# Attention, V's key spans of a unit: six transfers, alternately to the lower and the upper half of the partitions, in place of two

## The reference

```python
def _attn_ref(q, k, v):                  # batch 4, heads 8, seq 576, head_dim 64
    # 1: q, k, v averaged over groups of 4 tokens, full softmax attention on the 144 averages,
    #    each result repeated for its 4 tokens
    mask = np.abs(pos[:, None] - pos[None, :]) < factor        # factor = 4
    scores = np.where(mask, scale * np.matmul(q, k.transpose(0, 1, 3, 2)), -1000000000.0)
    out_local = np.matmul(softmax(scores), v)                  # 2: the seven nearest keys
    return out_up + out_local
def _moe_ref(x, w_in, w_out):            # 512 -> 2048 -> 512
    h = x @ w_in
    return (h * np.tanh(softplus(h))) @ w_out
def _moe2_ref(x, w_in, w_out, g_ln):     # 512 -> 1024 -> 512
    return (layernorm(h * softmax(h)) * g_ln) @ w_out          # h = x @ w_in
```

## Time and profile before

| | us |
|---|---|
| median of 3 runs | 689.77 |
| lowest and highest | 688.67, 690.86 |
| the profiled execution, first to last instruction | 686.9 |
| attention (start to the first product of the first feed-forward stage, L913) | 86 |

### The profile page before, as it was taken

One profiled execution on the slowest core, in us unless ns is written; L12 is line 12 of the kernel. 1 busy time (PEld: TensorE's weight loads), 2 busy tenths in 40 slices (PEclk: granted clock), 3 DMA queues, 4 the chain that ended last, 5 costly groups with the idle time before them and its releaser, 6 DMA issues.

```text
span 686.9 us, 12938 instructions
## 1 busy us (share of the span) xinstructions
PE 667.5 (97%) x5002; PEld 573.1 (83%) x5002; DVE 425.9 (62%) x747; ACT 326.0 (47%) x687; POOL 284.2 (41%) x342
## 2 busy tenths in 40 slices
PE   6998899999999999999999999999999999999998
PEld 5777778888999989989899988888778888888886
DVE  7998759555765557555544412555788566766671
ACT  5998773233543446543443211137464454535441
POOL 6999713020694636645000000576435543354100
PEclk9999999999999999999999999999999999999999
DMA  8999692000000000000100001012100000000001
GB/s 259 247 262 262 157 336 114 0 1 1 0 1 1 1 1 1 1 1 1 62 1 2 1 0 35 27 31 63 31 17 16 31 32 31 8 25 31 32 16 46
DMA packets 26085, 37.52 MB, mean 55 GB/s; under 512 B 2484, under 2 KB 12714, under 8 KB 26026
## 3 DMA queue, kind: packets, MB, share of 16 engines
q1 hardware_dynamic: 26026, 36.71, 18.0%
HBM read 31.98 MB, written 4.72 MB: 53 GB/s over the span
## 4 chain that ended last, share of the span: by engine, by line
PE 89%; POOL 3%; DVE 2%; issue 2%; ACT 1%; DMA 1%; SPq 0%; POOLq 0%; DVEq 0%
PE psum L961 29%; PE psum L913 16%; PE psum L1074 13%; PE psum L1051 12%; PE psum L947 12%; PE psum L1060 2%; PE psum L813 1%; POOL prob L676 1%; PE psum L845 1%; PE psum L893 1%; DVE so L1768 1%; PE psum L832 1%; POOL half_qk L649 1%; DMA qkT<-kT_dram 1%; POOL half_v L659 1%
## 5 line engine op out<-in xcount | busy, mean ns | idle before, releaser
L961 PE MATMUL psum<-ghi,whi 128*128 128x512 f32 (+1 forms) x320 | 118.2, 370 | 0.0
L961 PE MATMUL psum<-glo,whi 128*128 128x512 f32 (+1 forms) x320 | 118.1, 369 | 0.0
L961 PE MATMUL psum<-ghi,wlo 128*128 128x512 f32 (+1 forms) x320 | 117.7, 368 | 0.0
L1210 ACT ACTIVATE g_sb<-psum 128x512 f32<-128x512 f32 (+1 forms) x48 | 25.3, 527 | 135.5 <-PE psum L913 134.7
L1586 DVE CAST ghi<-g_sb 128x512 fp32r<-128x512 f32 (+1 forms) x48 | 24.0, 500 | 101.8 <-PE psum L961 86.7
L913 PE MATMUL psum<-xhi,whi 128*128 128x512 f32 (+1 forms) x256 | 85.6, 365 | 0.5 <-ACT g_sb L1210 0.3
L1591 DVE TENSOR_TENSOR glo<-g_sb,ghi 128x512 fp32r<-128x512 f32 (+1 forms) x80 | 66.3, 829 | 19.6 <-ACT ghi L1236 17.9
L961 PEld LDWEIGHTS psum<-ghi,wlo 128*128 128x128 f32 x320 | 60.3, 189 | 10.2
L961 PEld LDWEIGHTS psum<-ghi,whi 128*128 128x128 f32 x320 | 60.5, 189 | 9.8 <-issue 0.4
L913 PE MATMUL psum<-xlo,whi 128*128 128x512 f32 (+1 forms) x192 | 68.0, 354 | 0.0
L961 PEld LDWEIGHTS psum<-glo,whi 128*128 128x128 f32 x320 | 60.5, 189 | 8.9
(11 more groups left out here) (175 smaller groups left out, 1618.7 us busy)
## 6 DMA issues: line engine op xcount, KB each, us to landing
wraw<-w_dram SPq DMA_DIRECT2D x12, 512.0 KB, 7.5
vw<-v_dram SPq DMA_DIRECT2D x30, 160.0 KB
qkT<-qT_dram SPq DMA_DIRECT2D x16, 288.0 KB, 4.0
qkT<-kT_dram SPq DMA_DIRECT2D x16, 288.0 KB, 5.7
out_dram<-ob SPq DMA_DIRECT2D x18, 256.0 KB, 2.0
v<-v_dram SPq DMA_DIRECT2D x16, 256.0 KB, 5.8
wraw<-w_dram SPq DMA_DIRECT2D x16, 256.0 KB, 6.8
b<-w_dram SPq DMA_DIRECT2D x4, 512.0 KB, 4.3
```

What stands on the lines that cost most here:

```text
L961: ins = nc.tensor.matmul(psum[:, YB + m, 0:size], a[:, w], b[:, (t * F1 + f) % GR, 0:size], start=(f == 0 and n == 0), stop=(f == F1 - 1 a ...
L1210: nc.scalar.activation(g_sb[:, f % HR, 0:size], psum[:, HB1 + f % HB, 0:size], ACT.Mish).then_inc(g_ok, 1)
```

## The change

The spans of a unit are loaded in groups (0, 2), (2, 4), (4, 5) of i, and in each group first for jp = 0, then for jp = 1: six transfers of 64, 64, 64, 64, 32 and 32 KB in place of two of 160 KB. Bytes, rows and their addresses stay the same. Unit 0's piece L534 stays; the rest of its group has then one span. Unit 15's last span is loaded as 48 rows and 9 rows in place of 57. window_loads counts six for each unit.

```diff
         def window_loads(u):
-            return 2 * (u // 2 + 1) + (1 if u % 2 == 0 or u == UNITS - 1 else 0)
+            return 2 * len(GROUPS) * (u // 2 + 1) + (1 if u % 2 == 0 or u == UNITS - 1 else 0)
+
+        GROUPS = ((0, 2), (2, 4), (4, NP))
...
-                for jp in range(2):
-                    i0, i1 = 0, NP
-                    if u == 0 and jp == 0:
-                        sp.dma_start(vw[SHIFT:KW, par, 0, :], v_u[0:KW - SHIFT]).then_inc(ld_vw[par], 16)
-                        i0 = 1
-                    if u == UNITS - 1 and jp == 1:
-                        i1 = NP - 1
-                        k0 = window(i1, 1)
-                        sp.dma_start(vw[KW:KW + SEQ - k0, par, i1, :], v_u[k0:SEQ]).then_inc(ld_vw[par], 16)
-                    src = bass.AP(v_u.tensor, v_u.offset + window(i0, jp) * P,
-                                  [[P, KW], [PSTEP * P, i1 - i0], [1, P]])
-                    sp.dma_start(vw[jp * KW:(jp + 1) * KW, par, i0:i1, :], src).then_inc(ld_vw[par], 16)
+                for i0, i1 in GROUPS:
+                    for jp in range(2):
+                        first, rows = i0, KW
+                        if u == 0 and (i0, jp) == (0, 0):
+                            sp.dma_start(vw[SHIFT:KW, par, 0, :], v_u[0:KW - SHIFT]).then_inc(ld_vw[par], 16)
+                            first = 1
+                        if u == UNITS - 1 and (i1, jp) == (NP, 1):
+                            rows = 48
+                            k0 = window(i0, 1) + rows
+                            sp.dma_start(vw[KW + rows:KW + rows + SEQ - k0, par, i0, :], v_u[k0:SEQ])\
+                              .then_inc(ld_vw[par], 16)
+                        src = bass.AP(v_u.tensor, v_u.offset + window(first, jp) * P,
+                                      [[P, rows], [PSTEP * P, i1 - first], [1, P]])
+                        sp.dma_start(vw[jp * KW:jp * KW + rows, par, first:i1, :], src).then_inc(ld_vw[par], 16)
```

## The result

The kernel after takes 714.08 us, the median of six runs (712.98 to 715.5); the kernel before, beside it on the same chip, 689.22 us (685.37 to 692.5). The ratio is 1.0365, with an interval of 1.0344 to 1.0386: slower by 25 us. I had forecast slower by 5 us, with 703 as the upper end of the range.

A forecast was written before the change was run, and what follows sets the result against it. SP's queue was taken to bound the attention: +6.1 us for later unit 12 values, -1.3 coming back, +4.8 in sum, so the span goes from 686.9 to 691.7 and the time to 694.6 us; range 686.8 to 703.

The forecast's parts named there:

- What bounds the changed kernel: Attention, before 86 us: SP's queue never waits and sets the pace; unit 12's values begin 6.1 us later.
- The room of 1.1 us a stage: SP's queue waits 14.7 us in thirteen stages before the change; four more issues per unit must fit there.
- the price of an issue: Spans on SP's queue: 0.51 us per two-span issue, 0.47 for a one-span one; 3.0 us a unit, at most 3.8.
- The lengthened issues: SP's queue: issues lengthened while a 16 KB instruction packet is in flight, 0.7 us a stage, bounds nothing and 1.2.
- The sum of the queue: Start, spans, rest of stages, lengthened issues and two weight pieces: unit 12's span issues end at 79.5 us.
- What hides a part: Transfers land 5.8 us after issue where 2.0 do alone; issues some 3 us later land at the same time.
- What comes back: TensorE's 2.41 us stall in unit 12's values partly goes with less crowded DMA engines: 1.3 us back, bounds 0 and 3.5.
- No cost: Unit 15's extra issue, first weights behind it, semaphore counts cost nothing; DMA engines nothing for four more transfers, bound 0.1 us a unit.
- Hidden: Rival, chance 0.24: SP's queue just keeps up, 4.85 us a stage against 4.83; no change, 689.8 us.
- Faster: Rival, chance 0.18: finer alternation of halves eases the DMA engines, 3 us gained, 686.8; needs two-span issues under 0.5 us.
- Slower by more: Rival, chance 0.12: a two-span issue costs as much as a five-span one, 10.4 us more, 705.
- its second way: Within slower by more: a TensorE that waits in each unit may get the lower clock of 1.2 GHz oftener.

The follow-up runs named there:

- the merged q and k: q and k of a unit loaded in one transfer: 710.32 us on the kernel after, 690.7 us on the kernel before.
- the kernel cut by rows: Kernel before, units 1 to 14 loading spans in four transfers, 48 then 16 rows of five spans per half: 687.33 us, ratio 0.9978.
- the two series beside TensorE: In two transfer-only kernels without attention, 64 issues beside TensorE's small products: two lengthened issues each, 1.59 and 1.79 us, then 1.55 and 1.70 us.
- the two series without TensorE: Same transfer-only kernels, 64 issues with TensorE idle; in the first kernel none was longer than 0.442 us.
- the kernel with the early weights: Kernel after, first weight pieces issued in stages 3 to 6 in place of 13 to 16: 708.62 us, ratio 1.0271.

## Why the prediction was wrong

**What bounds the changed kernel**, SP's queue, was right. The room of 1.1 us a stage agrees with what the experiments found: 0.6 us more fit in (four issues of 48 and 16 rows), 1.3 us more did not (four of 64 rows, +5 us).

**The step that failed is the price of an issue.** I bounded the two-span issue of 64 rows by a transfer of two pieces on 128 rows, 0.47, and by the five-span issue, 0.63, and took the lower one "since a pair of pieces is nearer to two than to five"; I gave the one-span issue the price of k and v. Both assume that pieces make the price. At 64 rows they hardly do (0.60, 0.61 and 0.62 us for one, two and five): what the five-span issue had and q, k, v and the weights had not was its 64 rows. It was a row of the trace with the same number of rows as the new transfers, and it held the right price, 0.60 to 0.63, for one span as well as for five. So 3.0 us a unit should have been 3.9, beyond even my upper end of 3.8, since I had kept one-span issues cheap there too. Over 13 units that is 11.7 us, the largest part of the miss.

**The load behind a 64-row issue** is dearer too. v behind spans takes 0.58 us, not 0.43; the merged q and k behind v, or behind vt, takes 0.58 as well, so in that kernel there is more to it than the 64 rows, and I can't say what. The trace of before had such rows: the weights directly behind the spans, 0.61 us at 68.18, and v in the two stages in which it stands there without being lengthened, of which this is one:

```profile
19.15 0.61 SPq L559 DMA_DIRECT2D v<-v_dram  x1
```

Behind a weight piece v takes 0.43 (59.41 in the earlier trace rows), and in the kernel cut by rows the weight piece itself does, behind spans of 16 rows (at 61.13). So the prediction also misread a row: it has 0.61 for v behind a weight load, where 0.43 stands, and 0.61 is v behind the spans. It is 0.15 us in each of the ten stages in which v follows the spans, 1.5 us.

**The lengthened issues** were right: I took 0.7 us a stage, and they come to some 9.4 us in twelve stages, 0.78. That the instruction fetch lengthens them had rested on a coincidence in time; the two series beside TensorE make it firmer, since their four lengthened issues stand within 0.2 us of the four packets, and the two series without TensorE have neither. It is still a coincidence in time and no more.

**The sum of the queue** said 79.5 us for the end of unit 12's issues and it was 95.35. Of the 15.9 us, 11.7 + 1.5 + 1.0 have their names above; 0.6 is a queue that reached unit 0 0.2 us later and unit 0's seventh transfer, L537, which the sum left out; for 1.1 I have no row. Landing took 2.8 us, not 2.3.

**What hides a part** was right: v lands 3.3 us after its issue (median) in place of 5.8, and the queue's delay of 24.6 us at unit 12's issue is only 22.4 at its values.

**What comes back,** 1.3 us, did not show: the stall of 2.41 us is gone from its place, but TensorE now waits 21.5 us in ten pieces for spans. What that stall was isn't settled, and I didn't try it.

**No cost** was right for unit 15's tail and for the DMA engines (twice as many transfers in the row cut, nothing lost). **It was wrong for the first weights.** I looked at those behind the last stage and not at the pieces within stages 13 to 16, which stand in the same queue behind the spans. The last of them was issued at 102.57 and its wait held ScalarE for 6.36 us, behind it pprobT, and TensorE for 5.40. TensorE, busy for 2.8 of the 8 us from 99 to 107, then got a mean granted clock of 0.82, so a part of the time at the lower of its two levels, 1.2 GHz. From unit 13's values to unit 15's it is busy all the time in both kernels, with 156 products before and 160 after:

```profile
83.90:97.50 13.60, 13.60 (x156) 10.95 (x154) 6.49 (x11) 9.58 (x22) 3.02 (x3) 1.00 0.76 259
```

16.40 us at 0.82 are 13.4 us at full clock, near the 13.60 of before and the 13.4 of the kernel with the early weights: the clock costs 2.8 us there. With 1.6 us by which unit 13 is later than unit 12, that is some 4.3 us behind the queue's own delay. Moving the pieces gave 5.5 us back.

**Put together:** the 691.7 us that I had for the span, + 15.9 for the queue, + 0.5 for landing, + 1.3 that didn't come back, + 4.3 at the end, are 713.7; the profiled execution spans 713.6. The sum closes mostly because its terms are read from the same two traces; what stands on experiments is the price of an issue, the saving on the queue and the late weights.

**The rivals.** *Hidden* fell: the queue's waits are down to 1.7 us. *Faster* fell by its own condition, a two-span issue under 0.5 us; whether the alternation does the DMA engines any good was not tried where the queue has room. *Slower by more*, to which I gave 0.12, was the case, with its price of a two-span issue right ("costs as much as the five-span one") and its second way, the lower clock, present as well, though behind the attention and not in it. Its 705 was too low by the one-span issues, the load behind, the weights and what did not come back. The Trainium skill, "DMA: Bandwidth & Descriptors", section "Issuing engines are not separate DMA queues", has the sequencer's part small beside the transfer; for these transfers the trace says the opposite, 0.65 us of queue for 64 KB that take an estimated 0.26 us at 254 GB/s.

## What to carry to other kernels

A queue that issues transfers is an engine with its own busy time, although the page gives it no column: add up its issues and its waits before cutting a transfer into pieces, and everything else that stands in it, the next stage's weights included, goes late with it. Price a new transfer by a row that has the same number of partitions first, and then the same pieces; and where two bounds lie on either side of the decision (here 1.1 us of room), ask which property each of them shares with the new form before choosing between them. Where the queue has room, four cheap transfers cost no more than two; where it had none, the 0.3 us a stage taken off it came back whole.

## What of the hardware was not expected

- A transfer of exactly 64 rows holds SP's queue for 0.60 us, 0.17 more than the dearest of 128, 120, 112, 96, 80, 72, 60, 56, 52, 48, 40, 32, 24 and 16 rows of one piece (0.33 to 0.43).
- At 64 rows one, two and five pieces cost the same within 0.03 us; at 128 rows they cost 0.43, 0.47 and 0.53, and five pieces more still once some transfers are under way.
- Where a 16 KB packet of the instruction queue moves, the issue that it meets, or the next, takes 1.55 to 1.79 us in place of 0.43 (four of four).
- 61 rows, in a series of eight, hold the queue for 1.34 us at the median and 2.25 at most, while the first of them costs 0.28: there it seems to be the queue behind that is full, which I did not follow up.
